# Products of ones into an unread bank in four waits of TensorE: first score, first expert rows, last slot, first dense rows

## Chip, cores and metric

The kernel runs on one core of a Trainium2 chip. The metric is the device time of one execution in microseconds; lower is better.

## The reference

Three layers follow one another. Attention with a memory term, for 4 batches of 8 heads with 576 rows of 64:

```python
scores = scale * q @ k.T;  scores = where(causal, -1e9, scores)
a = exp(scores - max);  a /= a.sum(-1) + 1e-9;  local = a @ v
mem_out = (phi(q) @ M_prev) / (phi(q) @ z_prev + 1e-6)
x = g * mem_out + (1 - g) * local              # g = sigmoid(beta), per head
```

A mixture of 8 experts over 2304 tokens of 512, each token to the expert of its largest logit:

```python
e_idx = argmax(x @ w_gate)
out[mask] = gate_w * eom * (relu(x[mask] @ w1[e]) @ w2[e])     # w1[e] 512x1024, w2[e] 1024x512
```

And a dense layer: `h = x @ w_in; (h - tanh(h)) @ w_out`, with 2048 hidden columns. Inputs and outputs are float32.

## The kernel before

Every engine has its program written out by hand, with semaphores between them; the order on an engine is the order in the file. Most products are made of three: a value is split into a high part (fp32r) and the rest, and high x high, high x low and low x high are summed in PSUM.

**Attention** (1.3 to some 279 us) runs over 8 pairs of heads and 5 row tiles of 128 each. For each tile TensorE makes the scores (`score`, L1152 to L1166), VectorE the maxima (`nmx`, L832, L835), ScalarE the exponentials (`prob`, L584, L589); TensorE turns them (`turn`, L1217 to L1229), and VectorE and ScalarE copy them out (`pt`). `score` of a pair's first tile waits for `k_split` and `q_split`, raised by GpSimd after the low parts (L453, L463). ScalarE's L620, L626 and L628 make the high parts for the next pair. At the program's head TensorE waits for two semaphores, `c_pool` and `c_dve`, for GpSimd's constants (L429 to L447) and a mask of VectorE. The matrix of ones `onesb` is the fifth of these memsets; it is used by `count`.

**Routing**: `count` (L1200 to L1207) counts the tokens of each expert. VectorE then makes a table of 25 slots of 128 rows (`table`, L1007 to L1027), and its last step raises `r_table`. GpSimd scatters the rows of x to `x_sorted` by indirect DMAs; SyncE fills the gaps with zeros and, when all have landed, loads the slots' rows into `xin` (`load_x`, L393). TensorE waits for `r_table` behind its last `count`, since it reads from the table which weights a slot uses; only then does it come to `turn_in`.

**Experts** (to 620 us): `turn_in` (L1345) turns a slot's rows (4 transposes), VectorE splits them (`xt_hi` L1045, `xt_lo` L1047), `up` makes 24 products of 512 columns into `s_ps[0]` (L1356 to L1358), VectorE applies the relu (`hid`, L1052), `turn_hid` turns the result (8 transposes, L1378) into `s_ps[1]`, VectorE splits it (L1058, L1061), and `down` makes 24 products (L1369 to L1371). In the loop, `up` of a slot, `turn_in` of the next and `down` of the slot before stand between, so that VectorE's steps are hidden; the last slot's `down` has nothing in between. VectorE copies the result to `y_sb` (L1067), and SyncE stores it to `y_sorted`.

**Dense layer** (to the end): GpSimd gathers the rows in token order (`yg`, L551), VectorE applies the gate (`gate_y`, L1088, semaphore `gated`). TensorE turns the first three tiles (L1439), ScalarE and VectorE split them (L784, L1111), and then `first` (12 products of 384 columns for each of 16 column tiles, L1414 to L1416) and `second` (L1428 to L1430) alternate over 6 blocks of 384 rows. ScalarE and VectorE make h - tanh(h) between them (L756 to L760, L1098 to L1106).

The eight PSUM banks are `s_ps[0][0]`, `s_ps[0][1]`, `s_ps[1][0]`, `s_ps[1][1]`, `t_ps[0]`, `t_ps[1]`, `o_ps[0]` and `o_ps[1]`.

Of the kernel before, what the change touches and what calls it, by code (L numbers as in the profile page):

```python
# [11 lines left out]
P = 128  # L12
# [14 lines left out]
MASKED = -1.0e30  # L27
SMALL = 0.046875 * 0.046875
RING = 5
XIN = 3  # L30
TABLE = SLOTS + XIN - 1
UNITS = 2 * E
# [26 lines left out]
def build(nc, qt, qt2, kt2, v, mz, beta, wgo, w1, w2, w_in, w_out, out):  # L59
    ctx = ExitStack()  # L60
    with ctx:
        place = [16512]

        def sb(name, shape, dt):
            size = 1
            for n in shape[1:]:
                size *= n
            size = -(-size * (2 if dt == BF16 else 4) // 32) * 32
            t = nc.alloc_sbuf_tensor_at(name, shape, dt, offset=place[0])
            place[0] += size  # L70
            return t

        def sem(name):
            return ctx.enter_context(nc.semaphore(name))
# [12 lines left out]
        onesb = sb("onesb", [P, P], BF16)  # L87
# [63 lines left out]

        ring = sb("ring", [P, RING, 2, CD * F], F32R)
        end_weights = place[0]
        unit_bytes = 2 * CD * F * 4

        def place_of(at):
            return early + at * unit_bytes

        assert attention_end <= place_of(RING - 2) + unit_bytes // 2
        ring1 = ring[:, :, :, :].rearrange("p r t (c f) -> p r t c f", c=CD)  # L160
# [12 lines left out]
        w_out_lo = sb("w_out_lo", [P, CFF, DM], F32R)  # L173
        assert place[0] == place_of(RING - 1)

# [6 lines left out]
        place[0] = end_weights  # L182
        xin = sb("xin", [P, XIN, DM], F32)
        xt_hi = sb("xt_hi", [P, CD, P], F32R)
# [5 lines left out]
        assert place[0] <= 229368  # L190
        place[0] = place_of(RING - 1)
        yg = sb("yg", [P, TT, DM], F32)
# [13 lines left out]
        def bank(name):  # L206
            return ctx.enter_context(nc.psum_tensor(name, [P, 512], F32))

        s2_ps = [ctx.enter_context(nc.psum_tensor(f"scores{p}", [P, 2, 512], F32)) for p in range(2)]
        s_ps = [[s2_ps[p][:, h, :] for h in range(2)] for p in range(2)]  # L210
# [8 lines left out]
        t_ps = [bank(f"turned{h}") for h in range(2)]  # L219
# [8 lines left out]

        c_pool, c_pool2, c_dve, c_dma, c_gate = sem("c_pool"), sem("c_pool2"), sem("c_dve"), sem("c_dma"), sem("c_gate")  # L230
        zero_out = sem("zero_out")
        k_in = [sem("k_in0"), sem("k_in1")]
        q2_in = [sem("q2_in0"), sem("q2_in1")]
# [12 lines left out]
        scattered, filled = sem("scattered"), sem("filled")  # L246
        xin_ok = [sem(f"xin_ok{r}") for r in range(XIN)]
        w_ok = [sem(f"w_ok{r}") for r in range(RING)]
        early_hi, part_hi, part_lo, x_hi, h_hi, wo_lo = (sem(n) for n in ("early_hi", "part_hi", "part_lo", "x_hi", "h_hi", "wo_lo"))
# [24 lines left out]
        def ring_at(k):  # L274
            return RING - 1 - k % RING

# [21 lines left out]
        def _(sp):  # L298
# [91 lines left out]
            def load_x(t, k):  # L390
                row = sp.value_load(table[0:1, 2, bass.ds(t, 1)], min_val=0, max_val=E * REG)
                sp.wait_ge(x_turned, t + 1)
                sp.dma_start(xin[:, k % XIN, :], xs[bass.ds(row, P), :]).then_inc(xin_ok[k % XIN], 16)  # L393

            def store_y(t, k):
                sp.wait_ge(y_ok, t + 2)
                sp.dma_start(ys[bass.ds(t * P, P), :], y_sb[:, k % 2, :]).then_inc(y_out[k % 2], 16)

            for k in range(XIN):
                load_x(k, k)  # L400
            with sp.Fori(0, (SLOTS - 1) // SPAN) as i:
                for k in range(1, SPAN + 1):
                    load_x(i * SPAN + (k + XIN - 1), k + XIN - 1)
                    store_y(i * SPAN + (k - 1), k - 1)
# [15 lines left out]
        def _(pool):  # L420
            steps = [0]

            def step(ins):
# [2 lines left out]
                ins.then_inc(pool_step, 1)  # L426
                pool.wait_ge(pool_step, steps[0])

            pool.memset(ident[:, :], 0.0)  # L429
            pool.memset(identb[:, :], 0.0)  # L430
            pool.memset(maskb[:, :], 0.0)
            pool.memset(trib[:, :], 0.0)
            pool.memset(onesb[:, :], 1.0)
            pool.memset(q_st[:, :, 0, S:S + D].bitcast(F32), 0.0)
            pool.memset(mz_sb[:, :, :, :], 0.0).then_inc(c_pool2, 1)
            step(pool.memset(zeros[:, :], 0.0))
# [694 lines left out]
        def _(pe):  # L1131
            pe.sem_inc(down_done, 1)
            pe.sem_inc(x_turned, XIN)
            pe.wait_ge(c_pool, 2)
            pe.wait_ge(c_dve, 1)
            mm = pe.matmul

            def score(m):

# [202 lines left out]
            def turn_in(round, k):  # L1342
                pe.wait_ge(xin_ok[k % XIN], round * 16 + 16)
                for c in range(CD):
                    last = pe.transpose(t_ps[0][:, c * P:(c + 1) * P], xin[:, k % XIN, c * P:(c + 1) * P], ident[:, :])  # L1345
                last.then_inc(x_turned, 1)

            def up(t):
                e = pe.value_load(table[0:1, 0, bass.ds(t, 1)], min_val=0, max_val=E - 1)
                r = pe.value_load(table[0:1, 1, bass.ds(t, 1)], min_val=0, max_val=RING - 1)  # L1350
                pe.wait_ge(xt_ok, t + 1)
                pe.wait_ge(part_lo, e * 4 + 2)
                for j in range(2):
                    for c in range(CD):
                        h, l = (ring1[:, r, part, c, j * 512:(j + 1) * 512] for part in range(2))
                        mm(s_ps[0][j][:, :], xt_hi[:, c, :], h, start=c == 0, stop=False)  # L1356
                        mm(s_ps[0][j][:, :], xt_hi[:, c, :], l, start=False, stop=False)  # L1357
                        last = mm(s_ps[0][j][:, :], xt_lo[:, c, :], h, start=False, stop=c == CD - 1)  # L1358
                    last.then_inc(up_done, 1)

            def down(t):
                e = pe.value_load(table[0:1, 0, bass.ds(t, 1)], min_val=0, max_val=E - 1)
                r = pe.value_load(table[0:1, 3, bass.ds(t, 1)], min_val=0, max_val=RING - 1)
                pe.wait_ge(ht_ok, t * 2 + 2)
                pe.wait_ge(y_ok, t + 1)
                pe.wait_ge(part_lo, e * 4 + 4)
                for c in range(CF):
                    h, l = (ring2[:, r, part, c, :] for part in range(2))
                    mm(o_ps[0][:, :], hidt_hi[:, c, :], h, start=c == 0, stop=False)  # L1369
                    mm(o_ps[0][:, :], hidt_hi[:, c, :], l, start=False, stop=False)  # L1370
                    last = mm(o_ps[0][:, :], hidt_lo[:, c, :], h, start=False, stop=c == CF - 1)  # L1371
                last.then_inc(down_done, 1)

            def turn_hid(t):
                for j in range(2):
                    pe.wait_ge(relu_done, t * 2 + (j + 1))
                    for c in range(4):
                        last = pe.transpose(s_ps[1][j][:, c * P:(c + 1) * P], hid[:, (4 * j + c) * P:(4 * j + c + 1) * P], ident[:, :])  # L1378
                    last.then_inc(h_turned, 1)

            turn_in(0, 0)
            up(0)
            turn_in(0, 1)
            turn_hid(0)
            with pe.Fori(0, (SLOTS - 1) // SPAN) as i:
                for k in range(1, SPAN + 1):
                    t = i * SPAN + k
                    pe.wait_ge(relu_done, t * 2)
                    up(t)
                    turn_in(i * (SPAN // XIN) + (k + 1) // XIN, k + 1)  # L1390
                    down(i * SPAN + (k - 1))
                    turn_hid(t)
            down(SLOTS - 1)

# [23 lines left out]
            def second(t):  # L1419
# [13 lines left out]
                if t == BLOCKS * CFF - 1 - GRING:  # L1433
                    last.then_inc(g_free, 1)

            for r in range(TT):
                pe.wait_ge(gated, r + 1)
                for c in range(CD):
                    last = pe.transpose(first_turn[r][:, c * P:(c + 1) * P], yg[:, r, c * P:(c + 1) * P], ident[:, :])  # L1439
                last.then_inc(y_turned, 1 if r < TT - 1 else CD - r)  # L1440
# [46 lines left out]
```

## Time and profile before

| | |
|---|---|
| median of 3 runs | 1049.17 us (1047.05 to 1049.51) |
| the profiled execution | 1049.49 us, span 1047.7 us |
| mean granted clock of TensorE | 0.970 of full |
| TensorE matmul busy | 977.0 us, 93% |
| TensorE weight load busy | 813.5 us, 78% |
| VectorE, ScalarE, GpSimd busy | 647.6, 501.9, 473.3 us |

### The profile page before, as it was taken

What the parts mean: (1) busy time and instruction counts of PE and PEld (TensorE: products, weight loads), DVE (VectorE), ACT (ScalarE), POOL (GpSimd) and SP (SyncE); (2) the same over time, 40 slices, a digit from 0 to 9 for tenths busy, and PEclk for the clock granted to TensorE, in tenths of its full rate; (3) what the DMA queues carried; (4) which work ended last, traced back from release to release, by engine and by line L of the source; (5) the groups of instructions that cost most, each with busy time, mean ns of one, the idle gap of its engine ahead of it and who ended that gap; (6) DMA issues with size and microseconds to landing.
All of it is one profiled execution on the core that took longest, in us unless ns stands there. A gap on an engine that the chain in (4) does not pass through costs nothing.

```text
span 1047.7 us, 16574 instructions
## 1 busy us (share of the span) xinstructions
PE 977.0 (93%) x5377; PEld 813.5 (78%) x5378; DVE 647.6 (62%) x1242; ACT 501.9 (48%) x1042; POOL 473.3 (45%) x334
## 2 busy tenths in 40 slices
PE   3999989999549999999999969999999999999998
PEld 2667758577438888888888848899999999999997
DVE  3687776877624544444454426777777777777764
ACT  5777776776152120022112026556565565565554
POOL 5565585774589642067337045432232232322221
PEclk9999999999759999999999988999999999999999
DMA  9455565431576342155391111010010020100001
GB/s 207 123 150 138 155 197 140 134 100 33 194 263 253 134 151 100 42 214 184 120 365 47 49 44 38 1 31 31 1 61 1 1 61 1 31 31 1 31 1 31
DMA packets 50000, 101.81 MB, mean 97 GB/s; under 512 B 7312, under 2 KB 16528, under 8 KB 49424
## 3 DMA queue, kind: packets, MB, share of 16 engines
q1 hardware_dynamic: 33408, 54.85, 18.1%
q10 hardware_dynamic: 13616, 36.70, 9.7%
q0 software_dynamic: 2912, 9.44, 2.9%
q8 instruction: 36, 0.59, 0.2%
q14 instruction: 28, 0.23, 0.1%
HBM read 82.62 MB, written 18.35 MB: 96 GB/s over the span
## 4 chain that ended last, share of the span: by engine, by line
PE 76%; DVE 6%; DMA 2%; issue 1%; POOL 1%; ACT 0%; SPq 0%; DVEq 0%; POOLq 0%; ACTq 0%
PE scores L1414 6%; PE scores L1416 6%; PE scores L1415 6%; PE scores L1356 4%; PE average L1369 4%; PE scores L1358 4%; PE average L1371 4%; PE scores L1357 4%; PE average L1370 4%; PE average L1248 2%; PE average L1429 2%; PE mix L1430 2%; PE turned L1429 2%; PE average L1430 2%; PE turned L1430 2%; PE mix L1429 2%
## 5 line engine op out<-in xcount | busy, mean ns | idle before, releaser
L563 POOL TENSOR_TENSOR g_lo<-g,g_hi 128x384 fp32r<-128x384 f32 x96 | 97.7, 1018 | 279.0 <-ACT g_hi L764 278.5
L529 POOL TENSOR_TENSOR ring<-ring 128x2048 fp32r<-128x2048 f32 x30 | 137.2, 4605 | 109.8 <-ACT ring L706 106.0
L706 ACT ACTIVATE ring<-ring 128x2048 fp32r<-128x2048 f32 x30 | 55.7, 1907 | 183.5 <-PE average L1371 81.7
L1414 PE MATMUL scores<-yt_hi,w_in_hi 128*128 128x384 f32 x384 | 131.8, 343 | 1.5 <-DVE yt_lo L1111 1.5
L1416 PE MATMUL scores<-yt_hi,w_in_lo 128*128 128x384 f32 x384 | 130.1, 339 | 0.0
L1415 PE MATMUL scores<-yt_lo,w_in_hi 128*128 128x384 f32 x384 | 129.8, 338 | 0.0
L756 ACT ACTIVATE sq<-scores 128x384 f32<-128x384 f32 x96 | 47.2, 491 | 165.8 <-PE scores L1416 165.8
L1103 DVE COPY_PREDICATED ser<-big,th 128x384 f32<-128x384 int32 x96 | 118.9, 1239 | 3.3
L1098 DVE TENSOR_TENSOR ser<-ser,sq 128x384 f32<-128x384 f32 x96 | 55.9, 582 | 98.0 <-ACT ser L759 98.0
L589 ACT ACTIVATE prob<-scores,nmx 128x128 f32<-128x128 f32 (+3 forms) x128 | 66.3, 524 | 45.8 <-DVE nmx L835 45.4
L1356 PE MATMUL scores<-ring,xt_hi 128*128 x200 | 81.2, 406 | 3.1 <-DVE xt_lo L1047 3.1
L1369 PE MATMUL average<-ring,hidt_hi 128*128 x200 | 81.2, 406 | 2.5 <-DVE hidt_lo L1061 2.5
L1067 DVE COPY y_sb<-average 128x512 f32<-128x512 f32 x25 | 17.3, 691 | 103.0 <-PE average L1371 103.0
L1358 PE MATMUL scores<-ring,xt_lo 128*128 x200 | 79.2, 396 | 0.0
L1357 PE MATMUL scores<-ring,xt_hi 128*128 x200 | 79.0, 395 | 0.0
L1371 PE MATMUL average<-ring,hidt_lo 128*128 x200 | 78.9, 394 | 0.0
L1370 PE MATMUL average<-ring,hidt_hi 128*128 x200 | 78.5, 393 | 0.0
L1052 DVE TENSOR_SCALAR hid<-scores 128x512 f32<-128x512 f32 x50 | 34.6, 691 | 69.3 <-PE scores L1358 69.3
L1414 PEld LDWEIGHTS scores<-yt_hi,w_in_hi 128*128 128x128 f32 x384 | 72.9, 190 | 5.1 <-DVE yt_lo L1111 1.9
L1415 PEld LDWEIGHTS scores<-yt_lo,w_in_hi 128*128 128x128 f32 x384 | 72.8, 190 | 3.1
L1416 PEld LDWEIGHTS scores<-yt_hi,w_in_lo 128*128 128x128 f32 x384 | 72.6, 189 | 0.0
L835 DVE TENSOR_REDUCE nmx<-scores 128x2 f32<-128x256 f32 (+1 forms) x64 | 51.9, 810 | 32.3 <-PE scores L1155 21.9
(252 smaller groups left out, 2478.6 us busy)
## 6 DMA issues: line engine op xcount, KB each, us to landing
ring<-in_w ACTq DMA_DIRECT2D x13, 2048.0 KB, 9.1
q_sb<-in_qt SPq DMA_DIRECT2D x48, 288.0 KB, 4.4
k_sb<-in_kt SPq DMA_DIRECT2D x32, 288.0 KB, 4.2
xin<-x_sorted SPq DMA_DIRECT2D x27, 256.0 KB, 2.7
y_sorted<-y_sb SPq DMA_DIRECT2D x25, 256.0 KB, 2.1
v_sb<-in_v SPq DMA_DIRECT2D x16, 256.0 KB, 2.8
ring<-in_w SPq DMA_DIRECT2D x8, 512.0 KB, 4.2
w_out_sb<-in_w_out ACTq DMA_DIRECT2D x1, 4096.0 KB, 15.9
```

The costliest lines, as they stand in the source:

```text
L529: pool.tensor_tensor(ring[:, ring_at(k), 1, part], ring[:, ring_at(k), 1, part].bitcast(F32), ring[:, ring_at(k), 0, part].bitcast(F32), A ...
L563: pool.tensor_tensor(g_lo[:, t % GRING, :], g32[:, t % 2, :], g_hi[:, t % GRING, :].bitcast(F32), ALU.subtract).then_inc(g_lo_ok, 1)
L1103: dve.copy_predicated(ser[:, t % 2, :], big[:, t % 2, :].bitcast(I32), th[:, t % 2, :]).then_inc(f_step, 1)
L1356: mm(s_ps[0][j][:, :], xt_hi[:, c, :], h, start=c == 0, stop=False)
L1357: mm(s_ps[0][j][:, :], xt_hi[:, c, :], l, start=False, stop=False)
L1358: last = mm(s_ps[0][j][:, :], xt_lo[:, c, :], h, start=False, stop=c == CD - 1)
L1369: mm(o_ps[0][:, :], hidt_hi[:, c, :], h, start=c == 0, stop=False)
L1370: mm(o_ps[0][:, :], hidt_hi[:, c, :], l, start=False, stop=False)
L1371: last = mm(o_ps[0][:, :], hidt_lo[:, c, :], h, start=False, stop=c == CF - 1)
L1414: mm(ff_h(t), w_h, yt_hi[:, j % 2, c, :], start=c == 0, stop=False)
L1415: mm(ff_h(t), w_h, yt_lo[:, j % 2, c, :], start=False, stop=False)
L1416: last = mm(ff_h(t), w_l, yt_hi[:, j % 2, c, :], start=False, stop=c == CD - 1)
```

## The change

`onesb` is set first of GpSimd's constants, with a semaphore of its own, `c_ones`. A helper `idle_products(bank, count)` makes `count` matmuls of `onesb` (128x128 bf16) with itself broadcast to 512 columns. Each starts and stops its own sum in a bank that nobody reads until TensorE writes it anew. TensorE calls it at four places: 36 products into `t_ps[1]` at the program's head; 84 into `s_ps[1][1]` behind the wait for `r_table` and before the first `turn_in`; 9 into `s_ps[0][0]` before the last slot's `down`; and 30 into `s_ps[0][0]` before the first wait for `gated`. No result depends on them, and no wait is added but that for `c_ones`.

```diff
+AT_START, AT_EXPERTS, AT_LAST, AT_DENSE = 36, 84, 9, 30
...
+        c_ones = sem("c_ones")
...
+            pool.memset(onesb[:, :], 1.0).then_inc(c_ones, 1)
             pool.memset(ident[:, :], 0.0)
             pool.memset(identb[:, :], 0.0)
             pool.memset(maskb[:, :], 0.0)
             pool.memset(trib[:, :], 0.0)
-            pool.memset(onesb[:, :], 1.0)
...
             pe.sem_inc(x_turned, XIN)
+            mm = pe.matmul
+
+            def idle_products(bank, count):
+
+                for _ in range(count):
+                    mm(bank, onesb[:, :], onesb[:, None, :].to_broadcast([P, 4, P]), start=True, stop=True)
+
+            pe.wait_ge(c_ones, 1)
+            idle_products(t_ps[1][:, :], AT_START)
             pe.wait_ge(c_pool, 2)
             pe.wait_ge(c_dve, 1)
-            mm = pe.matmul
...
+            idle_products(s_ps[1][1], AT_EXPERTS)
             turn_in(0, 0)
             up(0)
             turn_in(0, 1)
...
                     down(i * SPAN + (k - 1))
                     turn_hid(t)
+            idle_products(s_ps[0][0], AT_LAST)
             down(SLOTS - 1)
...
+            idle_products(s_ps[0][0], AT_DENSE)
             for r in range(TT):
                 pe.wait_ge(gated, r + 1)
```

## Rows read from the trace of the kernel before

**Rows 1.** The page's chain that ended last: shares of the span by engine.
```profile
PE 76%; DVE 6%; DMA 2%; issue 1%; POOL 1%; ACT 0%; SPq 0%; DVEq 0%; POOLq 0%; ACTq 0%
```
**Rows 2.** Waits of TensorE: what waited, releaser, us in total, times, longest.
```profile
PE turned L1345 <- DMA xin<-x_sorted: 20.3, 1, 20.3
PE scores L1152 <- POOL q_st L463: 13.7, 1, 13.7
PE turned L1439 <- DVE yg L1088: 7.5, 1, 7.5
```
**Rows 3.** Timeline from the start: start us, us, engine, what [idle before, releaser].
```profile
1.27 0.20 POOL L433 MEMSET onesb<- 128x128 bf16 x1
...
14.37 0.41 PE L1153 MATMUL scores<-k_lo,q_st 128*128 128x128 f32 x1
...
14.58 0.44 PE L1157 MATMUL scores<-maskb,identb 128*128 128x256 bf16 x1
...
14.67 0.56 PE L1152 MATMUL scores<-k_hi,q_st 128*128 128x256 f32 x1
...
15.03 0.41 PE L1153 MATMUL scores<-k_lo,q_st 128*128 128x256 f32 x1
...
17.07 0.47 ACT L589 ACTIVATE prob<-scores,nmx 128x256 f32<-128x256 f32 x1 [0.75 <-DVE nmx L835]
...
19.54 0.58 ACT L589 ACTIVATE prob<-scores,nmx 128x384 f32<-128x384 f32 x1 [0.23 <-DVE nmx L835]
```
**Rows 4.** Windows of 1 us: length, busy PE, PEld, DVE, ACT, POOL, PEclk, DMA share, GB/s.
```profile
26.00:27.00 1.00, 0.91 (x5) 0.94 (x6) 0.60 (x1) 0.55 (x1) 0.00 (x0) 0.60 0.01 0
...
29.00:30.00 1.00, 1.00 (x7) 0.67 (x7) 0.93 (x4) 0.34 (x1) 0.50 (x1) 0.69 0.85 256
```
**Rows 5.** Windows of some 3.4 us: before a fall of the clock, and before none.
```profile
22.90:26.40 3.50, 1.59 (x10) 1.18 (x11) 2.26 (x3) 3.39 (x9) 2.62 (x1) 0.97 0.71 169
...
312.90:316.30 3.40, 2.00 (x12) 1.48 (x11) 3.37 (x7) 0.49 (x1) 3.40 (x2) 1.00 0.68 220
```
**Rows 6.** Timeline (and one window) of the first slot, and the last slot's down.
```profile
287.17 0.17 DVE L1027 TENSOR_SCALAR ends<-small_e 128x8 int32<-128x8 f32 x1
...
301.16 1.09 PE L1345 MATMUL turned<-ident,xin 128*128 128x128 f32 x4 [20.27 <-DMA xin<-x_sorted]
...
303.96 0.79 PE L1356 MATMUL scores<-ring,xt_hi 128*128 x1 [1.71 <-DVE xt_lo L1047]
...
304.55 0.63 PE L1357 MATMUL scores<-ring,xt_hi 128*128 x1
...
304.98 0.63 PE L1358 MATMUL scores<-ring,xt_lo 128*128 x1
...
309.00:310.00 1.00, 1.00 (x5) 0.82 (x4) 0.52 (x1) 0.33 (x1) 1.00 (x2) 0.75 0.01 4
...
311.88 0.39 PE L1358 MATMUL scores<-ring,xt_lo 128*128 x1
...
312.11 0.60 PE L1345 MATMUL turned<-ident,xin 128*128 128x128 f32 x4
...
612.60 0.49 PE L1369 MATMUL average<-ring,hidt_hi 128*128 x1 [2.50 <-DVE hidt_lo L1061]
```
**Rows 7.** Windows of 1 us in the last slot's down.
```profile
613.00:614.00 1.00, 1.00 (x5) 0.75 (x4) 0.00 (x0) 0.00 (x0) 1.00 (x1) 0.65 0.00 0
...
616.00:617.00 1.00, 1.00 (x4) 0.84 (x3) 0.00 (x0) 0.00 (x0) 0.00 (x0) 0.65 0.00 0
```
**Rows 8.** Timeline of the first dense rows.
```profile
627.48 1.12 PE L1439 MATMUL turned<-ident,yg 128*128 128x128 f32 x4 [7.54 <-DVE yg L1088]
...
630.40 1.11 PE L1439 MATMUL mix<-ident,yg 128*128 128x128 f32 x4 [0.30 <-DVE yg L1088]
...
633.05 0.69 PE L1414 MATMUL scores<-yt_hi,w_in_hi 128*128 128x384 f32 x1 [1.54 <-DVE yt_lo L1111]
...
637.30 0.49 ACT L756 ACTIVATE sq<-scores 128x384 f32<-128x384 f32 x1 [5.09 <-PE scores L1416]
```

## The prediction

> **What bounds the kernel now.** I read the page's chain first: work of TensorE makes 76% of it, so the end is set by TensorE's own work and by its few waits [rows 1]. Then the waits of TensorE, longest first: 20.3 us before the first expert rows, 13.7 us before the first score, 7.5 us before the first dense rows [rows 2], and 2.50 us before the last slot's second product [rows 6]. No engine is to be seen that could shorten these waits: they end on a DMA, on GpSimd's q_st, on the gated rows and on hidt_lo. So products that write an unread bank can't shorten them. What they can change is the clock of the work behind them. The windows show TensorE at half clock, 1.2 GHz, from 26.4 to 29.7 us [rows 4], from 613.35 to 616.65 us [rows 7] and until 309.25 us in the experts' first slot [rows 6]. At the start the page gives 1.00, but a matmul of 256 columns started 0.21 to 0.22 us after the one before (14.37, 14.58, 14.67, 15.03 us: three operations in 0.66 us) [rows 3], so that stretch ran at half clock too.
>
> **Price of one product.** It moves 512 columns of bf16. At half clock rows of 512 columns start 0.43 us apart (304.55, 304.98), at full clock 0.23 (311.88, 312.11) [rows 6]. That these are fp32r matters little: the bf16 matmul of 256 columns, also with a broadcast operand, fits its column count like its neighbours [rows 3]. 512 columns at 2.4 GHz are 0.213 us. I take 0.22 at full clock, bounds 0.213 and 0.23. How long the clock takes to rise under work: shortest 3.3 us (613.35 to 616.65 [rows 7]), then 5.3 us (303.96 to 309.25 [rows 6]) and somewhat over that in the first pair of heads. I take 5.1 us, 12 products; bounds 8 products (3.4 us) and 14 (6.0 us).
>
> **First score, 36 products.** The memset of onesb ended at 1.47 us as the fifth of its kind and now is the first [rows 3]; GpSimd does the same work in another order, so nothing else is later. The products start near 1.3 us and take 5.1 + 24 x 0.22 = 10.4 us: they end near 11.7 us, 2 us ahead of the first score at 13.69 (at the upper bounds 6.0 + 22 x 0.23 = 11.1 us, still in time). Cost nothing; the cover is the wait, which doesn't move. Gain: the scores then start at full clock. They halve, but ScalarE takes over: its idle time on the maxima was 0.75 and 0.23 us [rows 3], and behind them it has work without a gap. The maxima of the second tile stay behind a gate step of VectorE, so I give the early work 0.8 us, bounds 0.5 and 1.0. Then the second stretch at half clock, 26.4 to 29.7 [rows 4]. Ahead of it TensorE was busy for 1.59 of 3.50 us [rows 5]; with the next pair's scores 0.8 us earlier the same interval would hold some 2.3 us, more than the 2.00 of 3.40 us after which the clock stayed [rows 5]. If that fall goes, up to 3.3/2 = 1.65 us; if it only moves, nothing. I take 0.8. Sum -1.6, bounds -0.5 and -2.6. TensorE is nearly without waits in the rest of the attention, so this reaches the end.
>
> **First expert rows, 84 products.** This is the place that decides. The wait of 20.3 us [rows 2] is not all open to the products: they stand behind the wait for the table (r_table), which VectorE raises with its last table step, at 287.17 + 0.17 [rows 6]. From there to the first turn at 301.16 are 13.8 us. The products need 5.1 + 72 x 0.22 = 20.9 us and end at 308.2; bounds 3.4 + 76 x 0.213 = 19.6 (306.9) and 6.0 + 70 x 0.23 = 22.1 (309.4). The rows of x have long landed by then; turn_in, on the same queue, is 7 us late. Against it stands the full clock: from the first turn to the second slot's turn_in it was 312.11 - 301.16 = 10.95 us. Now: turn 0.60 (the turn at 312.11) + 1.7 for splitting (303.96 less the first turn's end at 302.25) + 24 x 0.23 = 5.5 [rows 6], 7.8 us in all. So the second turn_in starts at 308.2 + 7.8 = 316.0, +3.9 us, bounds +2.6 and +5.1. Every later expert step hangs on TensorE, which has no idle time from there to 610 us, so the 3.9 us stay. Nobody else profits: GpSimd and ScalarE only prepare weights that nobody waits for.
>
> Weighed against the Trainium skill, page "TensorE: Matmul & The Clock Gate", section "Back-to-back issue gap": it gives about 216 ns for a matmul of 512 columns by itself, near my 0.22, but about 131 ns in a sustained stream of loads and matmuls. By that figure the 84 products would end after 5.1 + 72 x 0.131 = 14.5 us, at 301.8, and this site would gain about 2.5 us. The trace disagrees: in its densest stream they start 0.23 us apart [rows 6].
>
> **Last slot, 9 products.** They follow turn_hid at full clock and take 9 x 0.22 = 2.0 us (bounds 1.9 and 2.1) of a wait of 2.50 us [rows 6], so they cost nothing. What goes is the fall at 613.35 with its 3.3 us at half clock [rows 7]: 8 products at 0.43 instead of 0.23, -1.6 us, bounds 0 (the clock falls all the same) and -1.6. The last slot's output is stored, gathered and gated in a chain, so all of it reaches the dense rows.
>
> **First dense rows, 30 products.** They take 30 x 0.22 = 6.6 us (6.9 at most), against a wait of 7.54 us [rows 8]; cost nothing. Then three turns with waits between them follow, to 633.05. The first and third, 1.12 and 1.11 us at half clock [rows 8], are on the chain; each would take 0.60 at full clock: bounds 0 and -1.0, I take -0.6. The first product of the dense layer is another matter. From the end of the products to 633 there are some 5.5 us with under 2.5 us of work. That is sparser than the interval before 26.4, after which the clock fell (1.59 of 3.50 us) [rows 5]. So I expect it to fall again between the turns, and the 12 matmuls to the first square at 637.30 [rows 8] to run at half clock as before: nothing gained. Held up, these 12 of 384 columns would take 0.16 us each instead of 0.32 (384 columns at 2.4 and at 1.2 GHz): 1.9 us less.
>
> **Sum.** 1047.7 - 1.6 + 3.9 - 1.6 - 0.6 = 1047.8 us of span. The profiled execution took 1049.49 us with its span of 1047.7, so 1.8 us lie around it: 1049.6 us, against a median of 1049.17.
>
> **Rivals.** (A) The forecast, 0.64: three small gains pay for one overrun. (B) The 84 products fit: that needs (301.16 - 287.34 - 5.1)/72 = 0.12 us for each, or a table wait that TensorE passes earlier. Then the site gives 10.95 - 7.8 = 3.1 us: 1047.7 - 1.6 - 3.1 - 1.6 - 0.6 + 1.8 = 1042.6 us. Against it: the 0.23 us of the rows and the program's order. 0.12; the page's stream figure belongs here. (C) Slower: products of constant ones don't raise the clock. It decides from the first wait on: 36 x 0.43 = 15.5 us would end at 16.8, 3.1 late, and 84 x 0.43 = 36.1 us at 323.4, 22.3 late, about 1049.5 + 25 = 1075 us. Against it: dense work at half clock always raised it in this trace. 0.04. (D) The clock holds through the turns of the first dense rows: 1.9 us less, 1047.7 us. 0.07. (E) The overrun at its upper bound (5.1), the start at its lower (-0.5, ScalarE being next), the clock of the last slot falling all the same, and nothing saved at the turns: 1047.7 - 0.5 + 5.1 + 1.8 = 1054.1 us. 0.13.
>
> Another rule of the Trainium skill, same page, Part 4, says that transposes don't count as activity of TensorE in the same way; by it (D) is all but excluded, since only turns lie between the products and the first dense rows. No row here shows that alone; it holds D's chance down and moves no time.
>
> **How the numbers follow.** Likeliest 1049.6 us. All favourable bounds with the overrun give 1047.7 - 2.6 + 2.6 - 1.6 - 1.0 - 1.9 + 1.8 = 1045.0; the unfavourable end is (E). The range is 1044.8 to 1054.0, leaving out B, C and some of the tails. A measurement of this kernel tells about 0.3%, 3.1 us, from no change. Faster than that: B, 0.12, half of D and a tail of A, 0.20 together. Slower: C, most of E, a tail of A, 0.17. Within: 0.63.
>
> **What would show it.** In the profile after: the 84 products start at 287 less some 1.6 us, and the first turn_in starts right behind them, its wait for x gone, some 5 us later than before; the granted clock is 1.00 over the first expert slot and over the last slot, and half again near 633 us; the second pair's first score comes 0.8 us earlier. A product much under 0.2 us, products ahead of the table, or full clock in the first dense tile would make the prediction wrong.

## The result and the profile after

Over 13 runs each, the changed kernel takes 1050.49 us in the median (1049.33 to 1051.88), the one before 1048.98 us (1046.94 to 1049.6): ratio 1.0019, 95% interval 1.0012 to 1.0027. That is slower by 1.5 to 2 us, less than the 0.3% that was taken as the bound of no change. The profiled execution took 1049.76 us with a span of 1047.9 us, 0.2 us above the span of before. So two spans that are nearly equal stand for medians that are 1.5 us apart: the profiled execution of before, with 1049.49 us, lay at the slow end of its kernel's runs, that of after, with 1049.76 us, near the fast end of its own. What goes with the 3 us by which executions of one program differ is told below, with the start.

The waits of TensorE after the change (what waited, releaser, us in total, times, longest):

```profile
PE scores L1141 <- DVE ends L1029: 6.5, 1, 6.5
...
PE scores L1162 <- POOL q_st L465: 1.8, 1, 1.8
PE scores L1366 <- DVE xt_lo L1049: 1.7, 1, 1.7
...
PE turned L1452 <- DVE yg L1090: 1.2, 1, 1.2
```

Three of the waits of [rows 2] are filled: 1.8 of 13.7 us are left before the first score, and 1.2 of 7.5 us before the first dense rows. The wait of 20.3 us on the DMA of x is gone altogether, and in its place stands a wait of 6.5 us for `ends`, the last step of the table. The products stand behind it. The timeline of TensorE shows the four groups (start us, us, what, in brackets the idle time before and its releaser):

```profile
1.05 10.79 PE L1141 MATMUL turned<-onesb 128*128 128x512 bf16 x36 [1.05 <-POOL onesb L431]
13.60 0.30 PE L1162 MATMUL scores<-k_hi,q_st 128*128 128x128 f32 x1 [1.76 <-POOL q_st L465]
...
24.63 0.44 PE L1162 MATMUL scores<-k_hi,q_st 128*128 128x128 f32 x1
...
285.39 20.65 PE L1141 MATMUL scores<-onesb 128*128 128x512 bf16 x84 [6.50 <-DVE ends L1029]
305.87 0.60 PE L1355 MATMUL turned<-ident,xin 128*128 128x128 f32 x4
308.18 0.49 PE L1366 MATMUL scores<-ring,xt_hi 128*128 x1 [1.71 <-DVE xt_lo L1049]
...
313.76 0.60 PE L1355 MATMUL turned<-ident,xin 128*128 128x128 f32 x4
...
611.58 2.11 PE L1141 MATMUL scores<-onesb 128*128 128x512 bf16 x9
614.27 0.49 PE L1379 MATMUL average<-ring,hidt_hi 128*128 x1 [0.58 <-DVE hidt_lo L1063]
...
619.84 6.65 PE L1141 MATMUL scores<-onesb 128*128 128x512 bf16 x30
627.66 0.66 PE L1452 MATMUL turned<-ident,yg 128*128 128x128 f32 x4 [1.17 <-DVE yg L1090]
...
630.39 0.66 PE L1452 MATMUL mix<-ident,yg 128*128 128x128 f32 x4 [0.61 <-DVE yg L1090]
...
632.59 0.69 PE L1426 MATMUL scores<-yt_hi,w_in_hi 128*128 128x384 f32 x1 [1.54 <-DVE yt_lo L1113]
```

The first turn of x (305.87) follows the 84 products at once, with no idle time before it: TensorE was late for the rows, not the rows for TensorE. The other three groups end before what they wait for. The windows show where the clock stood (length; busy us of PE, PEld, DVE, ACT, POOL; PEclk; DMA share; GB/s):

```profile
23.00:24.00 1.00, 0.52 (x6) 0.31 (x4) 0.61 (x2) 1.00 (x4) 1.00 (x1) 0.97 1.10 286
27.00:28.00 1.00, 1.00 (x8) 0.77 (x6) 0.90 (x4) 0.99 (x4) 0.00 (x0) 0.83 0.94 230
290.00:291.00 1.00, 1.00 (x6) 0.46 (x5) 0.00 (x0) 1.00 (x1) 1.00 (x1) 0.91 0.17 57
...
616.00:617.00 1.00, 1.00 (x6) 0.84 (x5) 0.00 (x0) 0.00 (x0) 0.13 (x1) 1.00 0.00 0
631.00:632.00 1.00, 0.05 (x1) 0.00 (x0) 0.29 (x2) 0.60 (x1) 0.68 (x1) 0.75 0.00 0
638.00:639.00 1.00, 1.00 (x7) 1.00 (x6) 0.73 (x2) 0.71 (x2) 0.00 (x0) 0.83 0.00 0
```

Half clock for a part x of a window of 1 us gives a mean of 1 - x/2. So the 0.97 in the window at 23 means that the clock fell at 23.94; it rose again at 27.34 (0.83). The stretch of [rows 4] is not gone, it has moved. At 290.18 the clock rose under the products, so the whole first slot ran at full clock, and the fall of [rows 7] is gone (1.00). At 631.5 it fell again, between the turns and the first dense products, and it rose at 638.34. In the kernel before it had risen at 637.18, 1.2 us earlier:

```profile
637.00:638.00 1.00, 1.00 (x6) 1.00 (x6) 0.00 (x0) 0.70 (x2) 0.00 (x0) 0.91 0.25 98
```

What each part cost, from marks in the two traces. The first two columns of numbers are us from the span's start, or the distance of two such marks:

| stretch | before | after | difference | forecast |
|---|---|---|---|---|
| start to the table's last step (its end) | 287.34 | 285.33 | -2.0 | -1.6 |
| from there to the second `turn_in` | 24.77 | 28.43 | +3.7 | +3.9 |
| second `turn_in` to the last slot's `down` | 300.49 | 300.51 | 0.0 | 0 |
| that `down` to its copy `y_sb` | 7.38 | 5.77 | -1.6 | -1.6 |
| the copy to the first dense product | 13.07 | 12.55 | -0.5 | -0.6 |
| that product to the end of the span | 414.65 | 415.31 | +0.7 | 0 |
| sum (span) | 1047.7 | 1047.9 | +0.2 | +0.1 |

(The copy starts at 619.98 us before and 620.04 after, the span ends with 1047.7 and 1047.9.)

### The profile page after: what moved, and what is told of

Same layout as the page of the kernel before. It is cut to its first block, busy times and chain, and to the rows that moved or that the text cites. A ratio compares the mean times of both kernels' runs of the same rounds, so it can differ in the third digit from the quotient of the medians.

```text
span 1047.9 us, 16891 instructions
## 1 busy us (share of the span) xinstructions
PE 1008.8 (96%) x5536; PEld 824.8 (79%) x5537; DVE 647.5 (62%) x1242; ACT 501.5 (48%) x1042; POOL 473.7 (45%) x334
## 4 chain that ended last, share of the span: by engine, by line
PE 71%; DVE 4%; POOL 3%; issue 1%; DMA 1%; ACTq 0%; ACT 0%; DVEq 0%; POOLq 0%
PE scores L1426 6%; PE scores L1428 6%; PE scores L1427 6%; PE average L1379 4%; PE average L1381 4%; PE average L1380 4%; PE scores L1368 4%; PE scores L1366 4%; PE scores L1367 4%; POOL ring L531 3%; PE average L1441 2%; PE mix L1442 2%; PE turned L1441 2%; PE average L1442 2%; PE turned L1442 2%; PE mix L1441 2%
## 5 line engine op out<-in xcount | busy, mean ns | idle before, releaser
L565 POOL TENSOR_TENSOR g_lo<-g,g_hi 128x384 fp32r<-128x384 f32 x96 | 97.8, 1019 | 279.6 <-ACT g_hi L766 279.1
```

What stands on the lines that cost most here:

```text
L565: pool.tensor_tensor(g_lo[:, t % GRING, :], g32[:, t % 2, :], g_hi[:, t % GRING, :].bitcast(F32), ALU.subtract).then_inc(g_lo_ok, 1)
```

## The experiments

Each kernel is the changed one with the edit shown. Ratios are against the kernel before, timed beside it on the same chip; they are not the quotient of the two medians, and can lie some 0.1% from it, so both are given. The median of before was 1048.04 us in the first four (29 runs), 1048.12 us in the next four (17 runs), 1049.07 us in the last four (11 runs).

**The sites one by one.** Four kernels, each with one site.

```diff
-AT_START, AT_EXPERTS, AT_LAST, AT_DENSE = 36, 84, 9, 30
+AT_START, AT_EXPERTS, AT_LAST, AT_DENSE = 36, 0, 0, 0     # start_alone
+AT_START, AT_EXPERTS, AT_LAST, AT_DENSE = 0, 84, 0, 0     # experts_alone
+AT_START, AT_EXPERTS, AT_LAST, AT_DENSE = 0, 0, 9, 0      # last_alone
+AT_START, AT_EXPERTS, AT_LAST, AT_DENSE = 0, 0, 0, 30     # dense_alone
```

> Only the 36 products at the program's head (the other three counts are 0). Theory (each site works by its own, the sum of the prediction): the second pair's first score comes 1.5 us earlier than in the kernel before, as in the trace after (24.63 against 26.09 us), and the end follows, -1.5 us. Rival (the start's gain is given back later, because the clock's falls in the attention only move): the first expert turn and the time are within 0.5 us of the kernel before.

> Only the 84 products before the first expert rows. Theory (they overrun the wait, since they stand behind the table): +3.6 us, the products end near 308 us and the first turn follows at once. Rival (the overrun is paid for by the full clock of the first slot and by slack in later waits): within 1 us of the kernel before.

> Only the 9 products before the last slot's down. Theory (the fall of the clock in it goes): -1.6 us up to the last down, no half clock between 610 and 620 us. Rival (the fall depends on how the execution lies to the chip's own clock of looking, so most timed runs save less): -0.8 us or less in the median.

> Only the 30 products before the first dense rows. Theory (the turns go faster, but the clock has fallen again when the dense rows begin): between -0.5 and +0.5 us, half clock at the first dense products. Rival (the clock holds through the turns in most runs, and the profiled one was an exception): -1.9 us or more.

| site alone | median us | ratio | 95% interval |
|---|---|---|---|
| start, 36 | 1047.9 | 0.9998 | 0.9988 to 1.0007 |
| experts, 84 | 1052.11 | 1.0033 | 1.0020 to 1.0046 |
| last, 9 | 1047.77 | 0.9995 | 0.9986 to 1.0004 |
| dense, 30 | 1049.0 | 1.0002 | 0.9993 to 1.0011 |

The experts' site alone costs 3.5 us (0.0033 of 1048): the theory's number. The dense site is worth nothing that can be told, as expected. The start and the last slot were both put too high: at most 1.3 and 1.5 us by their intervals, none for certain. There the rivals' numbers fit (within 0.5 us, and -0.8 us or less), not the theories'. By the ratios the four sites add up to +3.0 us, each known to about 1 us; the whole change measured +2.0 us. The profile of the start alone shows one reason why its gain is not always there:

```profile
1.05 9.39 PE L1141 MATMUL turned<-onesb 128*128 128x512 bf16 x36 [1.05 <-POOL onesb L431]
13.39 0.30 PE L1162 MATMUL scores<-k_hi,q_st 128*128 128x128 f32 x1 [2.96 <-POOL q_st L465]
```

```profile
14.00:15.00 1.00, 1.00 (x7) 0.66 (x5) 0.76 (x4) 0.81 (x2) 0.00 (x0) 0.64 1.14 314
17.00:18.00 1.00, 1.00 (x8) 0.69 (x7) 0.21 (x1) 1.00 (x2) 0.00 (x0) 0.66 0.98 212
```

The same 36 products took 9.39 us here and 10.79 us in the trace after. The clock rose earlier under them; so they were done earlier, 2.96 us were left instead of 1.76, and the clock fell again at 14.28 us, within the first scores, until 17.68. Products given by number don't fill a wait given by time. All eight profiles with products at the start agree: with 2.11 to 3.30 us left before the first score (six of them) the clock fell between 13.9 and 15.4 us, with 0.28 and 1.76 us it didn't. The second pair's first score came at 25.34 us, against 24.63 after and 26.09 before.

**A longer start.**

```diff
-AT_START, AT_EXPERTS, AT_LAST, AT_DENSE = 36, 84, 9, 30
+AT_START, AT_EXPERTS, AT_LAST, AT_DENSE = 42, 0, 0, 0
```

> Only the start, with 42 products instead of 36. With 36 alone the profiled execution had 3.0 us between the last product and the first score, and the clock fell within the scores (half from about 14.3 to 17.7 us); with all four sites it had 1.8 us and no fall. Theory (the gap decides): 6 more products leave at most 1.8 us, no fall in the first scores, and the median is about 0.8 us below the 36. Rival (the scores of the first pair hang on ScalarE and VectorE, the clock there hardly counts): the same median within 0.3 us.

Measured: 1048.36 us, ratio 0.9999 (0.9990 to 1.0008). In the profile the gap was filled, the first scores ran at full clock, and the second pair's first score came at 24.48 us, 1.6 us before that of the kernel before. But the clock fell at 23.96, and the median is no better. The rival was right about the time. Its reason isn't shown: the second pair's scores did come earlier, and the time was still not shorter.

```profile
1.05 12.10 PE L1141 MATMUL turned<-onesb 128*128 128x512 bf16 x42 [1.05 <-POOL onesb L431]
13.43 0.30 PE L1162 MATMUL scores<-k_hi,q_st 128*128 128x128 f32 x1 [0.28 <-POOL q_st L465]
```

```profile
23.00:24.00 1.00, 0.52 (x5) 0.36 (x4) 0.77 (x2) 1.00 (x4) 1.00 (x1) 0.98 1.06 267
27.00:28.00 1.00, 1.00 (x9) 0.83 (x10) 0.90 (x5) 0.84 (x4) 0.00 (x1) 0.81 0.99 244
```

**48 products before the experts.** Alone, and in the whole change.

```diff
-AT_START, AT_EXPERTS, AT_LAST, AT_DENSE = 36, 84, 9, 30
+AT_START, AT_EXPERTS, AT_LAST, AT_DENSE = 0, 48, 0, 0     # experts48_alone
+AT_START, AT_EXPERTS, AT_LAST, AT_DENSE = 36, 48, 9, 30   # all_experts48
```

> Only the site before the first expert rows, with 48 products instead of 84 (5.1 + 36 x 0.22 = 13.0 us, from 287.3 to 300.3). Theory (the 84 overrun by some 7 us, and the full clock behind them is worth about 3 us): -3 us against the kernel before, 6 to 7 us below the run with 84. Rival (the overrun costs little and the full clock gives little): within 1 us of the kernel before and 3.5 us or less below the run with 84.

> The change with 48 instead of 84 products before the first expert rows, the other three sites as they are. Theory: 6 to 7 us below the change, so -5 us against the kernel before. Rival (the sites don't add up, because the clock falls elsewhere): -3 us or less.

Measured alone: 1044.89 us, ratio 0.9971 (0.9960 to 0.9982), so -3.0 us; by the ratios that is 6.5 us below the 84 (the medians, of two chips, are 7.2 us apart). In the whole change: 1042.67 us, ratio 0.9952 (0.9939 to 0.9966), -5.0 us, as the theory said. The first expert rows of the kernel with 84 alone, and below it of the one with 48:

```profile
286.48 20.61 PE L1141 MATMUL scores<-onesb 128*128 128x512 bf16 x84 [6.51 <-DVE ends L1029]
306.93 0.60 PE L1355 MATMUL turned<-ident,xin 128*128 128x128 f32 x4
...
314.89 0.60 PE L1355 MATMUL turned<-ident,xin 128*128 128x128 f32 x4
```

```profile
285.54 12.74 PE L1141 MATMUL scores<-onesb 128*128 128x512 bf16 x48 [6.51 <-DVE ends L1029]
299.24 0.66 PE L1355 MATMUL turned<-ident,xin 128*128 128x128 f32 x4 [0.95 <-DMA xin<-x_sorted]
...
307.17 0.60 PE L1355 MATMUL turned<-ident,xin 128*128 128x128 f32 x4
```

From turn to turn both take 7.9 us; what differs is when the first starts, 20.45 us behind the first product or 13.70. With 48 the DMA is awaited again, for 0.95 us. So 36 products fewer give the same clock in the first slot, 6.75 us sooner behind the first product.

**Holding the clock into the dense rows.** Products also behind each of the three turns.

```diff
+AT_TURN = 3, 3, 6
...
-AT_START, AT_EXPERTS, AT_LAST, AT_DENSE = 36, 84, 9, 30
+AT_START, AT_EXPERTS, AT_LAST, AT_DENSE = 36, 48, 9, 30
...
                 last.then_inc(y_turned, 1 if r < TT - 1 else CD - r)
+                idle_products(s_ps[0][0], AT_TURN[r])
```

> As the run before, and 3, 3 and 6 more products behind the three turns of the first dense rows, in the waits that were seen there (0.80, 0.61 and 1.54 us in the trace after). Theory (the clock falls there because the turns alone are too little work): the clock stays at full into the dense products, 1.5 to 2 us below the run with 48 alone. Rival (VectorE is next in the first dense tiles, so a faster TensorE only waits): the clock stays, but less than 0.5 us.

> The same program as hold_dense48 (36, 48, 9, 30, and 3, 3, 6 behind the turns), once more beside the next three, so that they are compared on one chip. Expected: 1040 to 1041.5 us, no fall of the clock between 600 and 660 us.

Measured: 1040.66 us, ratio 0.9928 (0.9914 to 0.9941), and again 1040.19 us, ratio 0.9916 (0.9904 to 0.9929): the first of the two is 2.0 us under the whole change with 48 (1042.67), timed on the same chip. This is the fastest version found, 7.5 to 9 us under the kernel before. From the second of the two runs:

```profile
621.34 0.66 PE L1453 MATMUL turned<-ident,yg 128*128 128x128 f32 x4 [0.95 <-DVE yg L1091]
621.83 0.81 PE L1142 MATMUL scores<-onesb 128*128 128x512 bf16 x3
622.85 0.66 PE L1453 MATMUL average<-ident,yg 128*128 128x128 f32 x4 [0.21 <-DVE yg L1091]
...
624.84 1.46 PE L1142 MATMUL scores<-onesb 128*128 128x512 bf16 x6
626.55 0.44 PE L1427 MATMUL scores<-yt_hi,w_in_hi 128*128 128x384 f32 x1 [0.25 <-DVE yt_lo L1114]
```

Behind the first turn TensorE's waits shrink to 0.2 us each, and there is no half clock in the dense rows. Counted from the copy `y_sb` the three turns start after 7.40, 8.91 and 10.41 us, against 7.62, 9.08 and 10.35 in the changed kernel, so the products make none of them later by more than 0.06 us. From the first dense product to the end it is 412.65 us here, 414.65 us before and 415.31 us after. The held clock is worth 2.0 us there against the kernel before (1.4 to 2.7 us against the eight profiles with a half clock at that place, 414.1 to 415.3 us), and VectorE doesn't take it back. But the whole change with 48 also held the clock in its profiled execution (412.73 us), and the two profiled executions took the same, 1042.13 us and 1042.07 us. So the 2.0 us between the medians would have to come from other executions with 48, in which the clock falls there as it did in the changed kernel. That is argued, not shown.

**Taking sites away from that version, and holding the start too.** Timed on one chip together with the second run of it (1040.19 us).

```diff
-AT_START, AT_EXPERTS, AT_LAST, AT_DENSE = 36, 48, 9, 30
+AT_START, AT_EXPERTS, AT_LAST, AT_DENSE = 0, 48, 9, 30    # hold_no_start
+AT_START, AT_EXPERTS, AT_LAST, AT_DENSE = 36, 48, 0, 30   # hold_no_last
+AT_START, AT_EXPERTS, AT_LAST, AT_DENSE = 42, 48, 9, 30   # hold_both, with this in turn(m):
+                if m == 3:
+                    idle_products(o_ps[0][:, :], 5)
                 pe.wait_ge(exped, 2 * m + (2 if i == QT - 1 else 1))
...
                     last.then_inc(turned_a, 1)
+                    if m == 3:
+                        idle_products(o_ps[0][:, :], 2)
```

> The program before without the 36 products at the head. Theory (at the start the clock's rise is given back by a fall in the waits of the first pair, so the site is worth next to nothing): within 0.6 us of hold_dense48_again. Rival (it is worth the 1.5 us of the trace): 1.5 us slower.

> The same without the 9 products before the last slot's down. Theory (those alone save 1.53 us up to the dense turns, and the clock held behind keeps it): 1.0 to 1.6 us slower than hold_dense48_again. Rival (in most runs the clock doesn't fall there anyway): 0.5 us or less.

> hold_dense48 with 42 products at the head, and 5 and 2 more in the first pair's waits before and within its fourth turn (1.35 and 0.48 us in the trace). Theory (the fall near 24 to 26 us comes from these waits): no half clock in the first 30 us, the second pair's first score near 24.5 us and the third pair's near 51.5, 1 us or more below hold_dense48_again. Rival (falls later in the attention make up for it): the first 30 us as said, but the time within 0.5 us.

| kernel | median us | ratio | 95% interval |
|---|---|---|---|
| the version itself | 1040.19 | 0.9916 | 0.9904 to 0.9929 |
| without the start | 1042.3 | 0.9931 | 0.9918 to 0.9945 |
| without the last slot's | 1043.0 | 0.9949 | 0.9937 to 0.9961 |
| with both held | 1041.27 | 0.9928 | 0.9914 to 0.9942 |

Without the start it is 1.6 us slower by the ratios and 2.1 us by the medians, the rival's number, but the intervals overlap, and alone the start gave 0.2 us: its worth lies between nothing and some 2 us, and stays open. Without the last slot's products it is 2.8 us slower by the medians and 3.5 us by the ratios, with intervals that don't overlap. The two traces account for 1.8: from the last `down` to the first dense turn it takes 14.93 us instead of 13.17, with the clock down from 608.1 us to 611.5 (0.55 and 0.75 in the windows):

```profile
608.00:609.00 1.00, 0.69 (x2) 0.60 (x3) 0.03 (x1) 0.00 (x0) 1.00 (x1) 0.55 0.00 0
611.00:612.00 1.00, 1.00 (x5) 0.78 (x4) 0.00 (x0) 0.00 (x0) 0.00 (x0) 0.75 0.00 0
```

So the theory's 1.0 to 1.6 was too low, and the rival's 0.5 is out. The rest, 1 to 1.7 us, isn't seen in these traces; the intervals are wide enough to hold it. The profiled execution without these products was also the one of its six with the highest mean clock (0.985, the others 0.981 to 0.984), so the others may have lost more; no trace shows where.

Holding the start too kept the clock up near 25 us, and brought nothing:

```profile
24.00:28.00 4.00, 3.60 (x25) 2.52 (x23) 3.38 (x8) 3.12 (x12) 1.38 (x1) 1.00 0.67 166
174.00:175.00 1.00, 1.00 (x11) 0.94 (x11) 0.00 (x0) 0.44 (x2) 1.00 (x1) 0.68 1.06 272
```

The version without these products has a mean clock of 0.60 in the same four microseconds. The third pair's first score came at 52.23 instead of 53.24 us (51.5 expected). But here too the clock fell in the first scores (42 products were done 2.11 us early this time), and the second pair's first score came at 25.48 us, 1 us later than expected. Up to 270 us both profiles have four falls, this one at 13.9, 174.4, 198.3 and 263.1 us, the other at 14.5, 24.8, 239.8 and 263.7. So the theory's 1 us is out. That later falls make up for it, as the rival says, fits these two profiles; the median is 1.1 us higher, and the intervals leave room for no difference.

## Why the prediction was right, and where it wasn't

**The overrun.** This was the step that the forecast hung on, and it held by its own terms: the wait of the 84 products on the table, 6.5 us, took from the 20.3 us what the forecast said. The products took 20.5 us to the first turn (20.9 forecast), at 0.216 us each at full clock ((305.87 - 290.18) us for the 72.8 products left after 4.79 us at half clock). From the first turn to the second it took 7.9 us (7.8). Sum +3.7 by the marks, +3.5 us alone; the kernels with 48, -3.0 us alone, show that the number makes the loss.

**The start** came out as -2.0 us in the profile (-1.6 forecast) and as -0.2 us in the runs of it alone (-1.3 to +0.7). The -2.0 is taken from one pair of executions, and agrees with the forecast partly by luck. The second pair's first score came 1.46 us earlier, not 0.8. The forecast's second half was wrong: it gave 0.8 us for the fall near 26 us to go, since the earlier scores would fill the stretch before it. Of the eight profiles with the start's products six have a fall between 23.9 and 26 us. In the trace after it came at 23.94, before the second pair's first score (24.63), so there those scores were too late to prevent it.

It is the attention itself that spreads. The first product of the last `count`, the end of the attention, came at these times (us); beside them stands how often the clock fell before 270 us (behind that it fell once more in every profile, at 276.4 to 279.1 us; the half clock of the first scores without start products, which only the distances of the matmuls show, is not counted):

| without start products | falls | end | with them | falls | end |
|---|---|---|---|---|---|
| experts48_alone | 2 | 278.64 | after | 3 | 278.50 |
| last_alone | 3 | 279.32 | hold_no_last | 4 | 278.73 |
| experts_alone | 3 | 279.58 | start_alone | 4 | 278.95 |
| before | 4 | 280.50 | start42_alone | 4 | 279.00 |
| dense_alone | 4 | 280.56 | hold_dense48_again | 4 | 279.38 |
| hold_no_start | 4 | 280.76 | all_experts48 | 5 | 280.12 |
| | | | hold_dense48 | 5 | 280.43 |

(hold_both, with seven more products in the attention, has 4 falls and 279.05.) TensorE's instructions up to there are the same within the left column, and yet it spans 2.1 us, in the order of the falls. From one number of falls to the next the mean is 0.5 to 1.3 us later, in both columns. At the same number of falls the kernels with start products are earlier, by 1.0 us at three and 1.6 us at four in the mean. But they fall more often, 4.1 times in the mean against 3.3, first of all in the first scores, and what is left between the means of the columns is 0.6 us. So the start seems to shorten its own stretch, and further falls to take back a good part of it. The -2.0 us between before (4 falls) and after (3) holds one fall fewer. Thirteen profiles show this order; no experiment set the number of falls, so the cause is argued.

The same spread is in the timed runs: of 29 of the kernel before, 1046.95 to 1049.76 us, those up to 1048.43 us had mean clocks of 0.972 to 0.974, those from 1048.69 us on 0.969 or 0.970. With it, equal spans and unequal medians can go together.

**The last slot** was sized right in the trace (-1.6), and lies somewhere from 0.5 us (in the runs of it alone, whose interval holds nothing too) to 2.8 us (in the held version). A gain there may be given back in part when the clock is half at the first dense products: in last_alone, as after, it is 415.31 us from them to the end against 414.65; the other five profiles without the 9 products and with half clock there have 414.1 to 414.5.

**The first dense rows.** The clock fell again between the turns, as forecast. The turns at full clock saved 0.5 us (0.6), but the forecast of nothing behind them was short by 0.7 us: the dense products started at half clock in both, and it rose 5.75 us behind the first of them instead of 4.1. The chain there was also bounded by something the forecast left out: the third gathered tile. VectorE's gate on it starts at 629.85 (629.86 before) after 0.17 us of idle time on its DMA, so a faster first turn couldn't help; only the third one did.

**The rivals.** (B) and (C) are out: products take 0.216 us, not 0.12, and the clock rises under products of ones, after 4.8 us. The stream figure of the Trainium skill, page "TensorE: Matmul & The Clock Gate", section "Back-to-back issue gap", 131 ns for 512 columns, is not borne out by some 72 of them in a row, each with its own weight load, at 0.216 us; its other figure, about 216 ns, which it gives for a matmul by itself, is what the stream took. (D), the clock holding through the turns, had 0.07 and happened in one of the three profiled kernels that have the 30 products and none behind them (all_experts48, not after and dense_alone); so 0.07 was perhaps too low, and its price (1.9 us) was right: 2.0. The rule of the Trainium skill, same page, Part 4, that transposes don't count as activity in the same way, isn't decided here: with turns alone the clock fell in two profiles and held in the third. (E) didn't come together, but it is what the medians lean to: the start and the last slot near their lower bounds, and nothing saved at the turns.

**Readings.** Three readings of the clock in the prediction don't follow from its rows. A window mean of 0.60 is half clock for 0.8 of it, so the clock fell at 26.2, not 26.4; 0.65 twice gives 613.3 to 616.7, not 613.35 to 616.65; 0.75 gives 309.5, not 309.25. The shortest rise was therefore 3.4 us and the next 5.5 us. None of this changes the sum: it used 5.1 us, and the 84 products raised the clock after 4.8 us.

**The sum.** The forecast of 1049.6 us was 0.9 us below the median. The mechanism was right: 84 products stand behind the table's wait, overrun, and cost 3.5 us. The rest was partly luck. The forecast let three gains of 3.8 us pay for the overrun of 3.9 us; in the runs of one site each they are 0.5 us together. One reason why the trace of after fits the forecast better than the runs do is that this execution had one fall of the clock fewer in the attention than that of before. The terms mis-sized are the start (-0.2 instead of -1.6 us), the last slot (-0.5 instead of -1.6, in the held version more) and the dense rows (+0.2 instead of -0.6; in the trace +0.7 instead of 0 behind the turns).

## What to carry to other kernels

Before filling a wait with idle work, find where the filling stands in the engine's own order: a wait that the profile puts down to a DMA can hide an earlier wait of the same engine, and only the part behind that is open. Size the filling so that it ends in time even at its slow bound, since a product too many costs its full length on the path (36 too many cost 6.5 us here), while one too few costs only some clock. Gains by the clock must be measured over many executions: two profiles differed by 2.1 us here in a stretch whose instructions are the same. Before reading a gain from such a pair, count the falls of the clock in both.

## What the runs showed of the hardware that was not expected

- Products of ones raise the clock (4.8 us after the first of the 84), and the time it takes differs between executions: the same 36 products took 9.34 to 10.79 us in six profiles.
- A wait of 2.11 to 3.30 us right behind 9 to 11 us of dense products was followed by a fall of the clock within the next scores in all six profiles that have one; waits of 0.28 and 1.76 us were not. In those two the products also ended latest (13.2 and 11.8 us), so how long the wait was and when it began aren't told apart.
- With groups of three products between the turns, which leave some 0.2 us of idle time each, and six behind the last, the clock held into the dense rows in both profiles of that version and in those of its three variants. With the 30 products and turns alone it held in one of three.
- How often the clock falls in the attention differs between executions of the same instructions, 2 to 4 times before 270 us in the six profiles without start products, and its end moves with it, 278.64 to 280.76 us. A held start (0.60 to 1.00 in the window from 24 to 28 us) didn't lower the median.
